# Attention stage of a gated state kernel: readout one unit later, scores as quarter-array products

## The reference

```python
f = 1.0 / (1.0 + np.exp(-f_logit))
for t in range(S):
    state = f[:, :, t, :, None] * state + np.einsum('bhd,bhe->bhde', k[:, :, t], v[:, :, t])
    y[:, :, t] = np.einsum('bhd,bhde->bhe', q[:, :, t], state)
```

## Time and profile before

| | us |
|---|---|
| median of 3 runs | 972.83 (972.77 to 973.0) |
| profiled execution, its own time | 971.44 |
| its span | 969.6 |
| PE busy | 817.7 (84% of the span) |
| DVE busy | 429.4 (44%) |
| ACT busy | 375.9 (39%) |
| POOL busy | 326.7 (34%) |

### The profile page before, as it was taken

The page is one execution under the profiler, slowest core; times in us unless marked ns, Lnnn a source line. Parts: engine busy times, 40 slices in busy tenths (PEclk is TensorE's granted clock), DMA queues, the critical chain, the costliest instruction groups (busy, mean ns, idle before and its releaser), DMA issues.

```text
span 969.6 us, 15744 instructions
## 1 busy us (share of the span) xinstructions
PE 817.7 (84%) x5831; PEld 784.8 (81%) x5831; DVE 429.4 (44%) x830; ACT 375.9 (39%) x662; POOL 326.7 (34%) x248
## 2 busy tenths in 40 slices
PE   6999999602221399999999999999999999999995
PEld 4989888501221299999999999999999999999995
DVE  5777777486666424313423422432431432342331
ACT  4666666345543013323323322332331432332332
POOL 5677777460000307025223323412602612431001
PEclk9999999755555599999999999999999999999998
DMA  9999998211000102111111210300211211100000
GB/s 180 171 175 199 159 183 150 93 65 65 0 0 0 44 6 66 66 50 66 66 49 42 88 49 0 130 24 24 70 59 49 65 65 49 65 0 25 1 1 24
DMA packets 126802, 64.98 MB, mean 67 GB/s; under 512 B 102448, under 2 KB 119856, under 8 KB 126768
## 3 DMA queue, kind: packets, MB, share of 16 engines
q1 hardware_dynamic: 123696, 55.09, 25.1%
q0 software_dynamic: 3072, 9.44, 2.9%
HBM read 55.07 MB, written 9.44 MB: 67 GB/s over the span
## 4 chain that ended last, share of the span: by engine, by line
PE 82%; issue 8%; DVE 5%; ACT 2%; DMA 1%; DVEq 1%; SPq 0%; POOL 0%; ACTq 0%; POOLq 0%
PE psum L1278 21%; PE psum L1280 20%; PE psum L1279 20%; PE psum L1085 4%; PE psum L1136 3%; PE psum L1175 3%; PE psum L1182 3%; PE psum L1121 2%; PE psum L1236 1%; PE psum L1145 1%; PE psum L1164 1%; PE psum L1113 1%; PE psum L1288 1%; ACT junk_a L716 1%; PE psum L1251 1%
## 5 line engine op out<-in xcount | busy, mean ns | idle before, releaser
L1067 DVE SCALAR_TENSOR_TENSOR psum<-rg,psum 128x384 f32<-128x384 f32 x128 | 72.0, 563 | 155.2 <-ACT rg L750 155.2
L750 ACT ACTIVATE rg<-psum,three 128x384 f32<-128x384 f32 x128 | 74.5, 582 | 153.0 <-PE psum L1280 153.0
L1278 PE MATMUL psum<-yh,w_high 128*128 128x384 f32 x384 | 130.5, 340 | 1.0
L1280 PE MATMUL psum<-yh,w_low 128*128 128x384 f32 x384 | 128.5, 335 | 0.0
L1279 PE MATMUL psum<-yl,w_high 128*128 128x384 f32 x384 | 128.4, 334 | 0.0
L1280 PE MATMUL psum<-w_high,gl 128*128 128x384 f32 x384 | 128.3, 334 | 0.0
L1278 PE MATMUL psum<-w_high,gh 128*128 128x384 f32 x384 | 128.3, 334 | 0.0
L1279 PE MATMUL psum<-w_low,gh 128*128 128x384 f32 x384 | 128.3, 334 | 0.0
L608 POOL DMA_INDIRECT out_dram<-ys,ids x24 | 24.0, 1002 | 265.2 <-ACT ys L765 260.3
L1057 DVE SCALAR_TENSOR_TENSOR hl<-psum,hh 128x384 fp32r<-128x384 f32 x64 | 35.7, 558 | 166.8 <-ACT hh L740 150.9
L1070 DVE SCALAR_TENSOR_TENSOR gl<-psum,gh 128x384 fp32r<-128x384 f32 x128 | 71.4, 557 | 72.4 <-ACT gh L754 72.4
(11 more groups left out here) (180 smaller groups left out, 1725.9 us busy)
## 6 DMA issues: line engine op xcount, KB each, us to landing
raw<-in_moe_w_dram SPq DMA_DIRECT2D x16, 1536.0 KB, 6.4
f_in<-in_f_logit_dram SPq DMA_DIRECT2D x24, 192.0 KB, 4.2
k_in<-in_k_dram SPq DMA_DIRECT2D x24, 192.0 KB, 4.8
q_in<-in_q_dram SPq DMA_DIRECT2D x24, 192.0 KB, 5.1
v_in<-in_v_dram SPq DMA_DIRECT2D x24, 192.0 KB, 4.4
x_rows<-x_nat SPq DMA_DIRECT2D x24, 192.0 KB, 3.7
raw<-in_moe_w_in_dram SPq DMA_DIRECT2D x12, 256.0 KB, 4.4
raw<-in_moe_w_out_dram SPq DMA_DIRECT2D x12, 256.0 KB, 3.0
```

Source lines behind the costliest of these rows:

```text
L750: act.activation(rg[:, j % 2, :], banks[j % 3][:, 0:CAP], ACT.Relu, bias=three[:, 0:1]).then_inc(r_done, 1)
L1067: dve.scalar_tensor_tensor(out=bank, in0=rg[:, j % 2, :], scalar=6.0, in1=bank, op0=ALU.min, op1=ALU.mult).then_inc(gg_done, 1)
L1278: pe.matmul(bank, high, rhs_high, start=start, stop=False)
L1280: return pe.matmul(bank, low, rhs_high, start=False, stop=stop)
```

## The change

The readout of a unit (state read, values, copy of yT, transposes to x, logits) moves behind by one unit on each engine. The order of PE in a unit becomes: `turn_f`, key transposes, `turn_k`, `turn_q`, `turn_y` and `logits` of n - 2, scores of n, state read of n - 1, kv of n, values of n - 1. Each score product is cut in two along the columns of the array, so sixteen products of 64 rows by 64 columns take the place of eight of 64 by 128. On DVE the scan of n + 2 goes ahead of the mask, `scale_k` and `scale_q` come next, and then the state update, now of unit n - 1, then kv_sum of n, and logits of n - 2. v is loaded one step later in SP's list. The core of the diff:

```diff
# SP: load_v(n) split off load(n)
             for n in range(B, NT):
                 load(n)
                 if n > B:
-                    store_x(n - B - 1)
+                    load_v(n - 1)
+                if n > B + 1:
+                    store_x(n - B - 2)
                 load_chunk(n)
# ACT
-                if start_of(n) >= 1:
-                    x_out(n - 1, tt - (b == 0), (b - 1) % B)
+                if start_of(n) >= 2:
+                    x_out(n - 2, tt - (b < 2), (b - 2) % B)
                 if more:
                     decays(n + 2)
                 chunk_round(n, tt, b)
+                if start_of(n) >= 1:
+                    y_out(n - 1, (b - 1) % 2)
...
# DVE
             def unit(n, tt, b, more):
                 i = b % 2
+                if more:
+                    products(n + 2)
                 dve.wait_ge(a_ready, n + 1)
...
                 last.then_inc(masked, 1)
                 if more:
-                    products(n + 2)
+                    if more_state(tt):
+                        dve.wait_ge(kn_ready, n + 1)
+                    scale_k(n + 2, i)
+                if start_of(n) >= 1:
+                    dve.wait_ge(y_init, n)
+                if more or b < B - 1:
+                    scale_q(n + 1, 1 - i, (b + 1) % B)
+                if start_of(n) >= 1 and (more_state(tt) or b == 0):
+                    before = (b - 1) % B
+                    dve.wait_ge(kv_added, n)
+                    dve.tensor_tensor(state[:, before, :, 0:D], kv_sum[:, :, :],
+                                      by_pair(decay[:, before, :])[:, :, P - 1:P].broadcast_to([P, PAIRS, D]),
+                                      ALU.mult).then_inc(state_done, 1)
                 if more_state(tt):
                     dve.wait_ge(kv_ready, n + 1)
                     if start_of(n) >= 1:
                         dve.wait_ge(state_done, n)
                     dve.tensor_tensor(kv_sum[:, :, :], state[:, b, :, 0:D], kv_ps, ALU.add).then_inc(kv_added, 1)
-                if start_of(n) >= 1:
-                    logits_out(n - 1)
-                if more:
-                    if more_state(tt):
-                        dve.wait_ge(kn_ready, n + 1)
-                    scale_k(n + 2, i)
-                if more or b < B - 1:
-                    scale_q(n + 1, 1 - i, (b + 1) % B)
-                if more_state(tt):
-                    dve.wait_ge(y_init, n + 1)
-                    dve.wait_ge(kv_added, n + 1)
-                    dve.tensor_tensor(state[:, b, :, 0:D], kv_sum[:, :, :], ...
+                if start_of(n) >= 2:
+                    logits_out(n - 2)
# PE
                 if more_state(tt):
                     if start_of(n) >= 1:
                         pe.wait_ge(kv_added, n)
-                    if start_of(n) >= 2:
-                        pe.wait_ge(l_copied, n - 1)
+                    if start_of(n) >= 3:
+                        pe.wait_ge(l_copied, n - 2)
                     for g in range(PAIRS):
                         last = pe.transpose(kn_ps[:, P * g:P * g + P], k_sc[:, i, P * g:P * g + P], ident[:, :])
...
+                pe.wait_ge(q_scaled, n + 1)
+                pe.wait_ge(k_scaled, n + 1)
...
+                        for c in range(2):
+                            t = slice(HALF * c, HALF * c + HALF)
+                            at = P * g + HALF * c
+                            last = pe.matmul(a_ps[j][t, P * g:P * g + P], k_sc[r, i, at:at + HALF], q_sc[r, i, P * g:P * g + P],
+                                             start=True, stop=True)
+                last.then_inc(a_ready, 1)
+                if start_of(n) >= 1:
+                    state_read(n - 1, (b - 1) % B)
...
+                if start_of(n) >= 1:
+                    values(n - 1, tt - (b == 0), (b - 1) % B)
# PE, behind the last unit
+            turn_y(NT - 2, (B - 2) % 2)
+            logits(NT - 2, (B - 2) % 2)
+            state_read(NT - 1, B - 1)
+            values(NT - 1, TT - 1, B - 1)
+            turn_y(NT - 1, (B - 1) % 2)
+            logits(NT - 1, (B - 1) % 2)
             pe.wait_ge(steep_rows, 2)
             pe.matmul(banks[3][:, 0:1], ones[:, :], steep_sum[:, :], start=True, stop=True).then_inc(steep_summed, 1)
-            turn_y(NT - 1, (B - 1) % 2)
-            logits(NT - 1, (B - 1) % 2)
```

More of the change, by code:

```diff
@@ L417, in load, with load_v @@
                     sp.dma_start(dst[:, b, :, 0:D], src[b, :, tok, :].rearrange("h s d -> s h d")).then_inc(here[b], 16)
+            def load_v(n):
+                tt, b = n // B, n % B
                 if n >= B:
                     sp.wait_ge(y_ready, n - B + 1)
-                sp.dma_start(v_in[:, b, :, :], v[b, :, tok, :].rearrange("h s d -> s h d")).then_inc(loaded_v[b], 16)
+                sp.dma_start(v_in[:, b, :, :],
+                             v[b, :, tt * P:tt * P + P, :].rearrange("h s d -> s h d")).then_inc(loaded_v[b], 16)
             def load_chunk(n):
@@ L439, in _ @@
                 load(n)
+                load_v(n)
                 if n == 0:
@@ L450, in _ @@
                 if n > B:
-                    store_x(n - B - 1)
+                    load_v(n - 1)
+                if n > B + 1:
+                    store_x(n - B - 2)
                 load_chunk(n)
-            for n in range(NT - B - 1, NT):
+            load_v(NT - 1)
+            for n in range(NT - B - 2, NT):
                 store_x(n)
@@ L668, in unit, with y_out @@
                 chunk_round(n, tt, b)
+                if start_of(n) >= 1:
+                    y_out(n - 1, (b - 1) % 2)
+            def y_out(n, i):
                 act.wait_ge(y_ready, n + 1)
@@ L671, in unit @@
                     act.wait_ge(l_ready, n - 1)
-                act.copy(yT[:, b % 2, :], yT_ps).then_inc(yT_copied, 1)
+                act.copy(yT[:, i, :], yT_ps).then_inc(yT_copied, 1)
             units(act, unit)
+            x_out(NT - 2, TT - 1, B - 2)
+            y_out(NT - 1, (B - 1) % 2)
             x_out(NT - 1, TT - 1, B - 1)
@@ L830, in unit @@
                     dve.tensor_tensor(kv_sum[:, :, :], state[:, b, :, 0:D], kv_ps, ALU.add).then_inc(kv_added, 1)
-                if start_of(n) >= 1:
-                    logits_out(n - 1)
-                if more:
-                    if more_state(tt):
-                        dve.wait_ge(kn_ready, n + 1)
-                    scale_k(n + 2, i)
-                if more or b < B - 1:
-                    scale_q(n + 1, 1 - i, (b + 1) % B)
-                if more_state(tt):
-                    dve.wait_ge(y_init, n + 1)
-                    dve.wait_ge(kv_added, n + 1)
-                    dve.tensor_tensor(state[:, b, :, 0:D], kv_sum[:, :, :],
-                                      by_pair(decay[:, b, :])[:, :, P - 1:P].broadcast_to([P, PAIRS, D]), ALU.mult).then_inc(state_done, 1)
+                if start_of(n) >= 2:
+                    logits_out(n - 2)
             units(dve, unit)
@@ L853, in _ @@
             dve.memset(head_of_row[HALF:P, 1:2], 1.0).then_inc(steep_rows, 1)
+            logits_out(NT - 2)
             set_up = [0]
@@ L1127, in unit @@
                     turn_f(n + 2, tt + b // 2, (b + 2) % B)
+                if more_state(tt):
+                    if start_of(n) >= 1:
+                        pe.wait_ge(kv_added, n)
+                    if start_of(n) >= 3:
+                        pe.wait_ge(l_copied, n - 2)
+                    for g in range(PAIRS):
+                        last = pe.transpose(kn_ps[:, P * g:P * g + P], k_sc[:, i, P * g:P * g + P], ident[:, :])
+                    last.then_inc(kn_ready, 1)
+                if more:
+                    turn_k(n + 2, tt + b // 2, (b + 2) % B)
+                if more or b < B - 1:
+                    turn_q(n + 1, tt + (b + 1) // B, (b + 1) % B)
+                if start_of(n) >= 2:
+                    turn_y(n - 2, i)
+                if more_state(tt):
+                    pe.wait_ge(kn_copied, n + 1)
+                elif b == 0:
+                    pe.wait_ge(kv_added, n)
+                if start_of(n) >= 2:
+                    logits(n - 2, i)
                 pe.wait_ge(q_scaled, n + 1)
@@ L1135, in unit @@
                         r = slice(HALF * j, HALF * j + HALF)
-                        last = pe.matmul(a_ps[j][:, P * g:P * g + P], k_sc[r, i, P * g:P * g + P], q_sc[r, i, P * g:P * g + P],
-                                         start=True, stop=True)
+                        for c in range(2):
[3 more added lines that the diff above has]
+                                             start=True, stop=True)
                 last.then_inc(a_ready, 1)
+                if start_of(n) >= 1:
+                    state_read(n - 1, (b - 1) % B)
                 if more_state(tt):
-                    if start_of(n) >= 1:
-                        pe.wait_ge(kv_added, n)
-                    if start_of(n) >= 2:
-                        pe.wait_ge(l_copied, n - 1)
[L1144 to L1160, removed]
```

(12 more changed lines are left out.)

## The result

| | before | after |
|---|---|---|
| median of the runs, us | 972.91 (972.77 to 974.21, 4 runs) | 996.27 (994.57 to 996.85, 4 runs) |
| ratio after to before | | 1.0237, 95% interval 1.0221 to 1.0253 |
| profiled execution: time, span | 971.44, 969.6 | 996.0, 994.1 |

What follows compares the result with a forecast made beforehand. PE was taken to bound the kernel, without gaps in attention. Loop +15.1, start 0, last four units -1.1, end +2.5, flag's product +0.3: together +16.8 on 971.4 gives 988.2, plus 1.4 makes 989.6 us, range 979 to 998.

Steps and rivals of the forecast that it cites:

- pairs only: Rival: in the scores group only two tiles work together, so scores cost 0.87 us more; 996 us; chance 0.12.
- Three changes of tiling off PE: PE's unit goes from six stretches of one tiling to three: 3 x 0.15 = 0.45 us less.
- Sixteen products at the cost of eight: PE's scores: four tiles work together at 0.11 us a step, 8 steps, 0.92 us for the group.
- The round: Key transposes, scores, mask, scale_k, scale_q, state update, kv_sum, logits_out, key transposes, closed by the shared PSUM bank: 7.9 us.
- the stand itself: DVE's state update, reading two SBUF tensors, stands still 0.76 us until POOL's decay lets go.
- The mean unit: An attention unit takes 7.9 us, 0.89 more than before; 17 intervals make +15.1 us.
- The start: First unit, three transposed groups ahead of the first scores, fewer behind: 0, bounds -1 and +2 us.
- The last four units: Without kv and such a round, two changes of tiling less each: 4 x 0.3 = -1.1 us.
- The end: From the last scores' start to the end of logits: 6.71 us before, 9.22 after, so +2.5.
- the flag's product: At attention's end it comes behind the last logits instead of ahead: +0.3 us, an estimate.
- Routing and experts: Stages behind attention: routing starts when the last logits are there, so attention's gain or loss passes on one to one.
- The other side: Rival: DVE reaches kv_sum and logits_out before PE's key transposes; -0.45 to -0.5 us per unit, 965; chance 0.05.

Runs made afterwards that it cites:

- f1: e1 with ACT in the order exp, copy of the turned keys, den: 969.38 us, ratio 0.9958.
- f2: f1 with eight score products of 64 by 128: 972.00 us, ratio 0.9988.
- e4: The changed kernel with the scores back as eight products of 64 by 128: 995.59 us, ratio 1.0237.
- e3: The changed kernel with decays(n + 2) ahead of x_out(n - 2) on ACT: 989.15 us, ratio 1.0164.
- h1: The changed kernel, its loop's state update reading the scores' PSUM bank instead of kv_sum in SBUF (wrong output): units of 7.27 us, one run.
- f4: f1 with the flag's product ahead of the last turn_y and unit 0's scores ahead of its transposes: 970.34 us, ratio 0.9969.
- e1: The changed kernel with two kv_sum buffers, kv_sum(n) and logits_out(n - 2) right behind the mask on DVE, state update last: 977.17 us, ratio 1.0038.
- e2: The changed kernel, one kv_sum buffer, with state update, kv_sum and logits_out between mask and scale_k on DVE: 979.30 us, ratio 1.0057.

## Why the prediction was right

- **The number, and luck in it.** 996.27 is inside the range of 979 to 998, but outside the 985 to 994 that the prediction gave this mechanism, and it is the very number of *pairs only*, a rival that the score group of 1.10 us rules out. The mechanism was found; that the range held owes something to the room left for the rivals. The miss is 7.7 us between the profiled executions and 6.6 between the medians, and it is taken apart below.
- **Three changes of tiling off PE, 0.45 to 0.5 per unit: right.** PE's list is 6.51 (f1), 7.00 minus 0.49. Of it 0.21 is the score products' part (f2).
- **Sixteen products at the cost of eight: right.** 0.92 to the next start in the changed kernel, 0.92 forecast; pairs only is out.
- **The round: right in place and size.** Forecast from the first key transpose K, and measured 101.25 to 109.14, in one unit, the shortest of the four kinds below: scores 2.71, 2.67; mask 3.85, 3.84; decay 5.87, 5.81; state update 6.26, 6.24; kv_sum 7.41, 7.40; next K 7.89, 7.89. "The state's release by POOL decides and not its own start" is what e4 shows, for the 0.03 that it puts it to; the way through turn_y, x_out and lnr is what e3 shows; the stand itself, 0.76 forecast, is 0.71 in h1.
- **The mean unit, 7.89 forecast, 8.01 measured: a little short.** In the four units of a turn of the hardware loop I find 7.97, 7.98, 7.92 and 8.20 again and again: three are 0.03 to 0.09 over the forecast, one 0.31. That the long one is a delay at the loop's edge, which a full PE hides (before and in f1 all four are equal), isn't tested. 17 x 0.12 = 2.1 us of the miss.
- **The start, 0 forecast: 1.1 too low.** The third scores come at 31.8 us of the span instead of 30.7, within the bounds given. The last four units -0.8 (forecast -1.1, where 4 x 0.3 is 1.2). The end is +2.6 in all, where +2.5 and +0.3 for the flag's product were forecast; the product costs nothing, as f4 against f1 shows.
- **Routing and experts, forecast at no change: the step that failed, and the largest part of the miss.** "What attention gains or loses passes on one to one" leaves out 4.4 of 24.5 us of span. 2.9 of it lie in routing (h2's trace, a longer code of PE with nothing else changed, has 2.8, its runs 1.8 to 2.6; the cause is open, see there), and 1.5 in the first expert, where the granted clock rises from the lower of its two levels to the upper later in this execution: in the first 5 us in which PE is busy without a gap, the granted clock is 0.79 before (336 to 341 us) and 0.50 after (359.1 to 364.1). First the row before, then the one after, from 9 us ahead of the first product:

```profile
326.00:346.00 20.00, 12.90 (x63) 12.53 (x64) 3.35 (x6) 2.92 (x6) 6.14 (x6) 0.70 0.21 59
```

```profile
349.10:369.10 20.00, 13.04 (x55) 12.67 (x56) 3.35 (x6) 2.91 (x6) 5.92 (x6) 0.62 0.21 60
```

  In none of the other traces is the first expert more than 0.3 longer than before, so this part belongs to the one execution.
- **The sum:** start 1.1, loop 17.2 (17 x 1.01), last four -0.8, end 2.6, routing 2.9, first expert 1.5: 24.5, as measured. Attention makes 20.1 of it, where 16.8 were forecast.
- **The other side was real, but not in this kernel.** The Trainium skill, TensorEngine Tiling (Array Packing), Key Properties, says that changing the tiling mode drains TensorE. This case agrees as soon as no wait stands on the bank: with three changes fewer, f1's unit is 0.49 us shorter than before (0.45 forecast for the changes, up to 0.05 for shorter steps), and f1 4 us faster.
- **My later misses**, e1 and e2: in both I had counted the bank's waits for DVE and not the one for ACT, `kn_copied` ahead of the logits, though it is in the same bank.

## What to carry to other kernels

An instruction that frees a shared PSUM bank belongs right behind the product it reads, however the rest of the list is turned; for each reordering, follow every wait on the bank, of all engines, once round until it comes back to itself, and compare that with the busiest engine's list. An operation of DVE with two operands in SBUF has two prices, alone and beside POOL, and when both hang on the same event it pays the same one every time: swapping two lines of a third engine can be worth 0.4 us a unit. Making one engine's code longer can cost time in a later stage, so compare the stages behind the one that was changed too.

## What the runs showed of the hardware that I had not expected

- PE code that isn't executed can cost time: 96 products in a branch not taken, 1.8 us by the medians (h2, ratio 1.0027, 1.0014 to 1.0039), with a stop of 1.1 us in the middle of eighteen transposes; 33 such products in f1 cost nothing (h3).
- Four tiles of 64 by 64 keep the pace of two: 32 records in 1.10 us, 16 of the state read in 1.05 to 1.09.
- DVE's state update, where it stood on POOL, ended 0.35 us (its own time alone) after a point 0.12 to 0.16 us ahead of the end of POOL's record, in each of some 110 updates of six traces (before, after, e1, e3, e4, f2). So the stand can be forecast to about 20 ns.
